# Attention output with the probabilities stationary instead of the values, in a fused attention and feed-forward kernel

## The chip, the cores and the metric

The program runs on one core of a Trainium2 chip. The metric is the device time of one execution in microseconds (us); lower is better. Three runs of the kernel before are given, and one more execution was taken by the hardware profiler.

## What is computed

The reference, cut to the part that the change touches; two feed-forward layers follow it (a layer norm, an up product to 2048 columns with relu, a down product back to 512 and a residual; then a mixing over tokens and the same again).

```python
batch, n_heads, seq, head_dim = (4, 8, 576, 64)
...
scores = scale * np.matmul(q, k.transpose(0, 1, 3, 2))
...
scores = np.where(causal, -1000000000.0, scores + np.minimum(bias, 0.0))
scores = scores - np.max(scores, axis=-1, keepdims=True)
attn = np.exp(scores)
attn = attn / (np.sum(attn, axis=-1, keepdims=True) + 1e-09)
return np.matmul(attn, v).astype(np.float32)
```

## The kernel before, in words

There are 32 heads (4 batches of 8), handled one after the other. The 576 queries of a head are 5 tiles of 128 rows, the last with 64; because of the causal mask tile i needs only the keys of tiles 0 to i. Every float32 operand of a product is held as a high and a low part, and the products of the parts are added up in PSUM.

For one head u the engines do this:

- TensorE transposes the loaded q, k and the last rows (L646 to L672), makes the scores of tile i (`scores`, L674), and transposes the probabilities of tile i, so that keys lie on partitions (`transpose_probs`, L696).
- VectorE adds the bias and takes the row maximum (L1141), ScalarE takes the exponential (L942). ScalarE then copies the transposed probabilities out as their high part (`probs_high`, L952), VectorE makes the low part (`probs_low`, L1156).
- GpSimd splits the values of the head into high and low halves that lie beside each other, 64 columns each, in `v2` (`split_values`, L574). It waits until TensorE is done with the values of the head before.
- `times_values` (L706) multiplies values and probabilities, one head late: in the turn of head u it works on head u-1. The values are stationary (128 columns: high and low half of each of the 64 value columns), the probabilities move. Part 0 covers queries 0 to 255 (4 matmuls), part 1 queries 256 to 575 (10 matmuls). The result lies in one bank, `ps_x`, with the 64 + 64 value columns on partitions. ScalarE copies the lower half out (`out_low`, L959), VectorE adds the halves (`out_sum`, L1163). Since the bank is shared, part 1 waits for the sum of part 0.
- `transpose_out` (L728) turns the sum back in 5 transposes, so that queries lie on partitions, and VectorE scales it by one over the row sum into `x_head` (`out_scale`, L1180). SyncE stores `x_head` to DRAM (`store_head`, L381).

The work comes in stages. Heads 0 to 10 run alone (`head_alone` on each engine; AHEAD is 11). After them 21 heads (11 to 31) run with blocks of the first feed-forward layer between their pieces: `head` with `fill(1)` to `fill(8)`, 4 heads to one block. The output of the last head is finished in the following quarter of a block (`last_output`). The rest of the span is feed-forward work alone.

The order on every engine is written out by hand; an engine runs its own list in order and waits on semaphores. Two lists matter here beside those above. On GpSimd, in the stage of the heads alone, `pair` (L589) has for every head u: `split_values`, then `split_weights` of weight pair u (L560, four operations of 128x512). On SyncE, `head_alone` (L394) has for every head u: the last rows of head u+2, the values of head u+1, the sums of head u+2, q of head u+3, `store_head` of head u-1, k of head u+3, and `next_weights` (L389), which loads weight pair u+1. There are two staging slots for weights, and pairs 0 and 1 are loaded ahead of the loop.

## Time and profile before

| | us |
|---|---|
| median of 3 runs | 1136.02 |
| lowest and highest of them | 1135.39, 1136.83 |
| span of the profiled execution (first to last instruction) | 1134.1 |

The profiled execution has no total time of its own beside its span; what lies around the span is at most the difference to the runs, 1.3 to 2.7 us. Instructions in the profile are named by engine, line of the kernel, and output and input tiles. PE is TensorE's matmuls and PEld its weight loads, DVE is VectorE, ACT ScalarE, POOL GpSimd, SP SyncE; SPq is SyncE issuing a DMA. Matmuls overlap, so what one costs in a stream is the distance from its start to the start of the next, and not its duration. In the stage of the heads alone some tiles share memory with others: `w_hi`, `w_lo` and `zt` in rows of L691, L723 and L1159 are the second buffers of the transposed probabilities and of q and k.

### The profile page before, as it was taken

The page shows a single profiled execution, that of the slowest core. Times are in us where ns is not written, and L with a number is a line of the kernel's source. Part 1 is how long each engine was busy: PE and PEld are TensorE (multiplying, and loading weights), DVE is VectorE, ACT ScalarE, POOL GpSimd, SP SyncE. Part 2 cuts the span into 40 slices and gives each one's busy share as a digit, 9 for nine tenths or more (in the row PEclk, how much of TensorE's full clock was granted, in tenths as well). Part 3 has the DMA queues.
Part 4 walks back from the last instruction along what each step waited for, and adds up shares of the span by engine and source line. Part 5 has one row for each costly group of instructions (what it writes and reads, how often), then busy time and mean ns, then how long its engine had stood idle before and what let it go on. Part 6 is the DMA issues. An engine that isn't in the chain of part 4 may idle for free.

```text
span 1134.1 us, 21431 instructions
## 1 busy us (share of the span) xinstructions
PE 1099.9 (97%) x7320; PEld 967.4 (85%) x7320; DVE 490.6 (43%) x1252; ACT 399.9 (35%) x1051; POOL 161.0 (14%) x183
## 2 busy tenths in 40 slices
PE   6887999999999999999999998999999999999998
PEld 5776888888888888889889787889898898898987
DVE  5999456566565565652231365321212212112121
ACT  5887445445454454441221244111111111111111
POOL 2776533010101010102100032000000000000000
PEclk9999999999999999999999999999999999999999
DMA  6667343313222323114301156003101101011010
GB/s 157 167 181 198 109 111 94 90 40 110 57 74 74 92 74 92 42 49 129 130 1 55 38 197 218 13 19 121 55 0 55 40 15 55 0 55 55 0 38 19
DMA packets 126184, 88.57 MB, mean 78 GB/s; under 512 B 87425, under 2 KB 99713, under 8 KB 126145
## 3 DMA queue, kind: packets, MB, share of 16 engines
q1 hardware_dynamic: 123584, 79.67, 23.9%
q0 software_dynamic: 2560, 8.39, 2.2%
q8 instruction: 23, 0.38, 0.1%
q14 instruction: 17, 0.13, 0.0%
HBM read 69.61 MB, written 18.42 MB: 78 GB/s over the span
## 4 chain that ended last, share of the span: by engine, by line
PE 91%; DMA 4%; SPq 2%; issue 1%; DVE 1%; ACT 1%; POOL 0%; DVEq 0%; ACTq 0%; POOLq 0%
PE ps_up L815 12%; PE ps_acc L832 12%; PE ps_up L816 12%; PE ps_up L817 11%; PE ps_acc L833 11%; PE ps_acc L834 11%; PE ps_x L723 4%; PE ps_s L691 4%; PE ps_pt L702 4%; DMA x_in<-u_dram 2%; PE ps_up L802 2%; PE ps_x L891 1%; DMA u_dram<-x_pair 1%; PE ps_x L733 1%; PE ps_x L653 1%
## 5 line engine op out<-in xcount | busy, mean ns | idle before, releaser
L815 PE MATMUL ps_up<-zt,w_hi 128*128 128x256 f32 x1152 | 333.2, 289 | 1.5 <-DVE zt L1273 1.0
L816 PE MATMUL ps_up<-zt,w_hi 128*128 128x256 f32 x1152 | 324.7, 282 | 0.0
L817 PE MATMUL ps_up<-zt,w_lo 128*128 128x256 f32 x1152 | 322.4, 280 | 0.0
L1278 DVE SCALAR_TENSOR_TENSOR h_lo<-ps_up,h_hi 128x256 fp32r<-128x256 f32 x288 | 122.2, 425 | 441.4 <-ACT h_hi L1029 440.8
L1029 ACT ACTIVATE h_hi<-ps_up 128x256 fp32r<-128x256 f32 x288 | 110.0, 382 | 494.1 <-PE ps_up L817 493.9
L832 PE MATMUL ps_acc<-w_hi,h_hi 128*128 128x512 f32 x576 | 237.1, 412 | 0.0
L815 PEld LDWEIGHTS ps_up<-zt,w_hi 128*128 128x128 f32 x1152 | 217.7, 189 | 15.0 <-DVE zt L1273 5.3
L833 PE MATMUL ps_acc<-w_lo,h_hi 128*128 128x512 f32 x576 | 227.1, 394 | 0.0
L834 PE MATMUL ps_acc<-w_hi,h_lo 128*128 128x512 f32 x576 | 227.1, 394 | 0.0
L816 PEld LDWEIGHTS ps_up<-zt,w_hi 128*128 128x128 f32 x1152 | 217.5, 189 | 7.4 <-issue 0.2
L817 PEld LDWEIGHTS ps_up<-zt,w_lo 128*128 128x128 f32 x1152 | 217.9, 189 | 0.0
L949 ACT ACTIVATE prob<-prob,neg_max 128x128 f32<-128x128 f32 (+4 forms) x160 | 96.8, 605 | 119.3 <-DVE neg_max L1152 119.3
L834 PEld LDWEIGHTS ps_acc<-w_hi,h_lo 128*128 128x128 f32 x576 | 108.4, 188 | 26.2
L832 PEld LDWEIGHTS ps_acc<-w_hi,h_hi 128*128 128x128 f32 x576 | 109.8, 191 | 13.3 <-issue 0.2
L833 PEld LDWEIGHTS ps_acc<-w_lo,h_hi 128*128 128x128 f32 x576 | 108.8, 189 | 13.9 <-issue 0.2
L1152 DVE CUSTOM_DVE_ANT_0 prob<-ps_s,ncum_b 128x128 f32<-128x128 f32 (+4 forms) x149 | 78.0, 524 | 52.4 <-PE ps_s L693 48.6
L702 PE MATMUL ps_pt<-ident_f,prob 128*128 128x128 f32 (+1 forms) x414 | 65.4, 266 | 11.4 <-ACT prob L949 11.4
L578 POOL TENSOR_TENSOR v<-v_raw,one 128x320 fp32r<-128x320 f32 x32 | 23.6, 737 | 284.6 <-PE ps_x L723 266.9
L1159 DVE TENSOR_TENSOR pt_lo<-ps_pt,pt_hi 128x128 fp32r<-128x128 f32 (+4 forms) x123 | 58.8, 478 | 7.2 <-ACT pt_hi L955 7.1
L955 ACT ACTIVATE pt_hi<-ps_pt 128x128 fp32r<-128x128 f32 (+4 forms) x123 | 52.9, 430 | 18.2 <-PE ps_pt L702 17.3
L702 PEld LDWEIGHTS ps_pt<-ident_f,prob 128*128 128x128 f32 (+1 forms) x414 | 41.0, 140 | 17.8 <-issue 12.9
L691 PE MATMUL ps_s<-k_hi,q 128*128 128x256 f32 (+4 forms) x146 | 51.8, 359 | 0.0
(138 smaller groups left out, 1209.0 us busy)
## 6 DMA issues: line engine op xcount, KB each, us to landing
ncum_b<-ncum_dram SPq DMA_DIRECT2D x32, 288.0 KB, 3.7
k_raw<-in_k SPq DMA_DIRECT2D x64, 128.0 KB, 2.7
stage<-in_moe_w_ch SPq DMA_DIRECT2D x32, 256.0 KB, 3.9
x_in<-x_dram SPq DMA_DIRECT2D x9, 512.0 KB, 3.6
x_res<-x_dram SPq DMA_DIRECT2D x9, 512.0 KB, 4.0
u_dram<-x_pair SPq DMA_DIRECT2D x2, 2304.0 KB, 10.9
x_in<-u_dram SPq DMA_DIRECT2D x9, 512.0 KB, 4.5
x_res<-u_dram SPq DMA_DIRECT2D x9, 512.0 KB, 3.7
```

The lines of the kernel that those rows point to most:

```text
L691: last = nc.tensor.matmul(bank, q2[:, i * P:(i + 1) * P], kk[:, lo:hi], start=(n == 0), stop=(n == 1 and not diag))
L702: last = nc.tensor.transpose(bank[:, c * r:(c + 1) * r], prob_of(p, i, alone)[0][0:r, c * P:(c + 1) * P], ident[0:r, 0:r])
L815: nc.tensor.matmul(up[j % 2][:, 0:BLK], w1_hi[:, j, c], zt_hi[:, c], start=(c == 0), stop=False)
L816: nc.tensor.matmul(up[j % 2][:, 0:BLK], w1_hi[:, j, c], zt_lo[:, c], start=False, stop=False)
L817: last = nc.tensor.matmul(up[j % 2][:, 0:BLK], w1_lo[:, j, c], zt_hi[:, c], start=False, stop=(c == KC - 1))
L832: nc.tensor.matmul(acc[t], h_hi[:, j % 2, cols], w2_hi[:, j], start=first, stop=False)
L833: nc.tensor.matmul(acc[t], h_hi[:, j % 2, cols], w2_lo[:, j], start=False, stop=False)
L834: last = nc.tensor.matmul(acc[t], h_lo[:, j % 2, cols], w2_hi[:, j], start=False, stop=final)
L949: nc.scalar.activation(at[:, 0:w], at[:, 0:w], ACT.Exp, bias=least, scale=-1.0, accum_out=row_sum[:, p, i:i + 1]).then_inc(exp_done, 1)
L1029: nc.scalar.activation(h_hi[:, j % 2], up[j % 2][:, 0:BLK], ACT.Relu).then_inc(L.h_hi_done, 1)
L1152: nc.vector.tensor_tensor_reduce(out=like(to[:, 0:w]), in0=scored, in1=like(ncum_b[p][:, 0:w]), scale=1.0, scalar=3.0e38, op0=ALU.add, op1 ...
L1278: nc.vector.scalar_tensor_tensor(out=h_lo[:, j % 2], in0=up[j % 2][:, 0:BLK], scalar=0.0, in1=h_hi[:, j % 2].bitcast(F32), op0=ALU.max, op ...
```

## The change

The two operands of the product change places. For query tile i and key tile c the transposed probabilities are stationary (`pt[:, c * ROW + i * P ...]`, 128 columns, 64 in the last tile) and the values move (128 columns). Tiles 0 to 2 are part 0, tiles 3 and 4 part 1. The queries now lie on partitions; VectorE adds the two halves, which lie beside each other in the free dimension, by `tensor_reduce` into `x_sum`, once in part 0 and twice in part 1; GpSimd scales `x_sum` into `x_head`. `out_low` and `transpose_out` are gone. GpSimd's list for a head u in the stage of the heads alone is now `split_values` (u), `split_weights` (u), `out_scale` (u-1); in the later heads it is `split_values` (u), `out_scale` (u-1), and then weights where there are any. The first `out_sum` of a head waits until the scaling of the head before is done with `x_sum`.

```diff
-PARTS = (0, 2 * P, S)
-MOST = max(PARTS[1], S - PARTS[1])
+OUT_TILES = ((0, 1, 2), (3, 4))
...
+            def out_scale(m, p):
+                u = 2 * m + p
+                pool.wait_ge(x_sum_done, 2 * u + 2)
+                pool.wait_ge(inv_done, u + 1)
+
+                waits_apart(pool, (x_stored, 32 * u))
+                pool.tensor_tensor(x_head[:], x_sum[:], inv_sum[:, p].unsqueeze(2).to_broadcast([P, QT, D]), ALU.mult)\
+                    .then_inc(x_head_done, 1)
...
                 for p in range(2):
                     split_values(m, p)
                     split_weights(2 * m + p, p, m)
+                    if not (isinstance(m, int) and m == 0 and p == 0):
+                        out_scale(*before(m, p))
...
                     split_values(*beside(n, i))
+                    out_scale(*before(*beside(n, i)))
                     for j in range(AHEAD + 2 * i, min(AHEAD + 2 * i + 2, JC)) if weights else ():
...
-                waits_apart(pe, (q_loaded, 16 * u + 16), (l_lo_done, u) if alone else (x_head_done, u - 1))
+                waits_apart(pe, (q_loaded, 16 * u + 16), (l_lo_done, u) if alone else (x_sum_done, 2 * (u - 1)))
...
-                begin, end = PARTS[a:a + 2]
-                tiles = -(-end // P)
-                for c in range(tiles):
-                    lo, hi = max(c * P, begin), end
-                    for pt in (pt_hi, pt_lo):
-                        last = nc.tensor.matmul(ps_x[:, lo - begin:end - begin], v2[:, c].rearrange("p a d -> p (a d)"),
-                                                pt[:, c * ROW + lo:c * ROW + hi], start=(c == 0 and pt is pt_hi),
-                                                stop=(c == tiles - 1 and pt is pt_lo))
-                last.then_inc(ot_done, 1)
-
-            def transpose_out(m, p):
...
+                wait(pe, x_sum_done, 2 * u + a)
+                for i in OUT_TILES[a]:
+                    r, at = rows(i), (i - OUT_TILES[a][0]) * P
+                    for c in range(i + 1):
+                        for pt in (pt_hi, pt_lo):
+                            last = nc.tensor.matmul(ps_x[0:r, at:at + P], pt[:, c * ROW + i * P:c * ROW + i * P + r],
+                                                    v2[:, c].rearrange("p a d -> p (a d)"), start=(c == 0 and pt is pt_hi),
+                                                    stop=(c == i and pt is pt_lo))
+                last.then_inc(out_done, 1)
...
-            def out_low(m, p, a):
-                act.wait_ge(ot_done, 2 * (2 * m + p) + a + 1)
-                n = PARTS[a + 1] - PARTS[a]
-                nc.scalar.activation(ot_low[:, 0:n], ps_x[D:2 * D, 0:n], ACT.Copy).then_inc(ot_low_done, 1)
...
             def out_sum(m, p, a):
                 u = 2 * m + p
-                dve.wait_ge(ot_low_done, 2 * u + a + 1)
+                dve.wait_ge(out_done, 2 * u + a + 1)
                 if a == 0:
 
-                    wait(dve, ox_done, u)
-                n = PARTS[a + 1] - PARTS[a]
-                nc.vector.tensor_tensor(ot_sum[:, PARTS[a]:PARTS[a + 1]], ps_x[0:D, 0:n], ot_low[:, 0:n], ALU.add)\
-                    .then_inc(ot_sum_done, 1)
+                    wait(dve, x_head_done, u)
+                first, n = OUT_TILES[a][0], len(OUT_TILES[a])
+                both = ps_x[:, 0:n * P].rearrange("p (t a d) -> p t d a", t=n, a=2)
+                if a == 0:
+                    last = nc.vector.tensor_reduce(x_sum[:, 0:n], both, mybir.AxisListType.X, ALU.add)
+                else:
+                    nc.vector.tensor_reduce(x_sum[:, first:QT - 1], both[:, 0:n - 1], mybir.AxisListType.X, ALU.add)
+                    last = nc.vector.tensor_reduce(x_sum[0:LAST, QT - 1:QT], both[0:LAST, n - 1:n], mybir.AxisListType.X, ALU.add)
+                last.then_inc(x_sum_done, 1)
...
-            def out_scale(m, p):
-                u = 2 * m + p
-                dve.wait_ge(ox_done, u + 1)
-                dve.wait_ge(inv_done, u + 1)
-
-                wait(dve, x_stored, 32 * u)
-                nc.vector.tensor_tensor(x_head[:], ps_x[:, 0:QT * D].rearrange("p (t d) -> p t d", d=D),
-                                        inv_sum[:, p].unsqueeze(2).to_broadcast([P, QT, D]), ALU.mult).then_inc(x_head_done, 1)
```

## Rows read from the trace of the kernel before

**Rows 1.** Windows: length, busy us of PE, PEld, DVE, ACT, POOL; clock, DMA, GB/s.

```profile
28.20:104.80 76.60, 66.25 (x543) 56.83 (x542) 72.08 (x218) 65.98 (x189) 55.63 (x54) 1.00 0.72 193
121.10:512.90 391.80, 391.78 (x2782) 343.63 (x2781) 229.66 (x632) 196.93 (x533) 60.76 (x67) 1.00 0.28 76
104.80:121.10 16.30, 11.62 (x76) 10.62 (x75) 10.10 (x28) 8.12 (x21) 7.26 (x7) 0.79 0.49 134
```

**Rows 2.** Timeline of PE, one later head: start, duration, line, tiles, shape.

```profile
284.85 0.36 PE L723 MATMUL ps_x<-pt_hi,v 128*128 128x256 f32 x1
...
285.34 0.45 PE L832 MATMUL ps_acc<-w_hi,h_hi 128*128 128x512 f32 x1
...
288.80 0.31 PE L723 MATMUL ps_x<-pt_hi,v 128*128 128x320 f32 x1
...
290.05 0.44 PE L702 MATMUL ps_pt<-ident_f,prob 128*128 128x128 f32 x2
...
292.08 0.40 PE L834 MATMUL ps_acc<-w_hi,h_lo 128*128 128x512 f32 x1
292.41 0.52 PE L733 MATMUL ps_x<-ident_f,ot_sum 64*128 64x64 f32 x5
292.86 0.55 PE L702 MATMUL ps_pt<-ident_f,prob 128*128 128x128 f32 x3
...
293.82 0.60 PE L653 MATMUL ps_x<-ident_f,q_raw 128*64 128x128 f32 x4
294.18 0.36 PE L815 MATMUL ps_up<-zt,w_hi 128*128 128x256 f32 x1
```

**Rows 3.** Timeline of PE's weight loads in the same head.

```profile
285.18 0.19 PEld L723 LDWEIGHTS ps_x<-pt_lo,v 128*128 128x128 f32 x1
285.29 0.19 PEld L832 LDWEIGHTS ps_acc<-w_hi,h_hi 128*128 128x128 f32 x1
```

**Rows 4.** Groups by line and shape: busy us, mean ns of one, idle before.

```profile
L578 POOL TENSOR_TENSOR v<-v_raw,one 128x320 fp32r<-128x320 f32 x32 | 23.6, 737 | 284.6 <-PE ps_x L723 266.9 <-DMA v_raw<-in_v 10.5 <-issue 7.2
...
L1152 DVE CUSTOM_DVE_ANT_0 prob<-ps_s,ncum_b 128x384 f32<-128x384 f32 x32 | 17.6, 550 | 0.0
...
L1186 DVE TENSOR_TENSOR x_head<-ps_x,inv_sum 128x320 f32<-128x320 f32 x32 | 15.6, 488 | 12.3 <-PE ps_x L733 12.3
L1170 DVE TENSOR_TENSOR ot_sum<-ps_x,ot_low 64x320 f32<-64x320 f32 x32 | 15.4, 481 | 15.2 <-ACT ot_low L962 15.0
...
L962 ACT ACTIVATE ot_low<-ps_x 64x320 f32<-64x320 f32 x32 | 13.9, 435 | 17.1 <-PE ps_x L723 16.5
```

**Rows 5.** Timeline of SP issuing, heads alone.

```profile
50.58 0.42 SPq L385 DMA_DIRECT2D x_dram<-x_head  x1
...
53.21 0.37 SPq L323 DMA_DIRECT2D stage<-in_moe_w_ch  x1
...
59.46 0.41 SPq L385 DMA_DIRECT2D x_dram<-x_head  x1
...
67.40 0.41 SPq L385 DMA_DIRECT2D x_dram<-x_head  x1
```

**Rows 6.** Waits of SP, 20 to 110 us: us in total, times, longest.

```profile
SPq L71 <- DVE x_head L1186: 0.4, 2, 0.2
```

**Rows 7.** Timeline of POOL, heads alone.

```profile
57.46 1.04 POOL L570 TENSOR_TENSOR w_hi<-stage,one 128x512 f32 x1 [2.33 <-DMA stage<-in_moe_w_ch]
...
62.45 0.72 POOL L578 TENSOR_TENSOR v<-v_raw,one 128x320 fp32r<-128x320 f32 x1
63.25 0.86 POOL L580 TENSOR_TENSOR v<-v_raw,v 128x320 fp32r<-128x320 f32 x1
```

**Rows 8.** Timelines of POOL and PE at the ends of the heads alone.

```profile
33.57 1.29 POOL L572 TENSOR_TENSOR w_lo<-stage,w_hi 128x512 fp32r<-128x512 f32 x1
...
104.52 0.28 PE L723 MATMUL ps_x<-w_lo,v 128*128 128x64 f32 x1
...
113.36 0.58 PE L815 MATMUL ps_up<-zt,w_hi 128*128 128x256 f32 x1 [0.96 <-DVE zt L1273]
```

More of the change, by code:

```diff
@@ L138, in chain_kernel @@
                               for name, w1 in (("pt_hi", w1_hi), ("pt_lo", w1_lo)))
-            ot_low = sbuf("ot_low", [D, MOST], F32, small)
-            ot_sum = sbuf("ot_sum", [D, SP_PAD], F32, small)
+            x_sum = sbuf("x_sum", [P, QT, D], F32, small)
             x_head = sbuf("x_head", [P, QT, D], F32, small)
@@ L609, in _ @@
             split_weights(AHEAD - 1, 0, AHEAD // 2)
+            out_scale(*before(AHEAD // 2, 0))
             group(0, weights=True)
@@ L613, in _ @@
             split_values(*LAST_HEAD)
+            out_scale(*before(*LAST_HEAD))
+            out_scale(*LAST_HEAD)
             pool.wait_ge(x_stored, 32 * HEADS)
@@ L712, in times_values @@
                     pe.wait_ge(v_split, u + 1)
-                    wait(pe, x_head_done, u)
-                else:
-                    pe.wait_ge(ot_sum_done, 2 * u + 1)
-                begin, end = PARTS[a:a + 2]
-                tiles = -(-end // P)
-                for c in range(tiles):
-                    lo, hi = max(c * P, begin), end
-                    for pt in (pt_hi, pt_lo):
-                        last = nc.tensor.matmul(ps_x[:, lo - begin:end - begin], v2[:, c].rearrange("p a d -> p (a d)"),
-                                                pt[:, c * ROW + lo:c * ROW + hi], start=(c == 0 and pt is pt_hi),
-                                                stop=(c == tiles - 1 and pt is pt_lo))
-                last.then_inc(ot_done, 1)
-            def transpose_out(m, p):
-                u = 2 * m + p
-                waits_apart(pe, (ot_sum_done, 2 * u + 2))
-                for t in range(QT):
-                    last = nc.tensor.transpose(ps_x[:, t * D:(t + 1) * D], ot_sum[:, t * P:(t + 1) * P], ident[0:D, 0:D])
-                last.then_inc(ox_done, 1)
+                    if not alone:
+                        pe.wait_ge(l_lo_done, u + 1)
+                wait(pe, x_sum_done, 2 * u + a)
[7 more added lines that the diff above has]
+                last.then_inc(out_done, 1)
             def head_alone(m, p, first=False, final=False):
@@ L752, in head_alone @@
                 transpose_probs(m, p, 3, True)
-                if not first:
-                    transpose_out(*before(m, p))
                 transpose_probs(m, p, 4, True)
@@ L773, in head @@
                 fill(4)
-                transpose_out(*before(m, p))
                 transpose_probs(m, p, 2, False)
@@ L858, in last_output @@
                     times_values(*LAST_HEAD, step, False)
-                else:
-                    transpose_out(*LAST_HEAD)
             def first_input():
@@ L957, in probs_high @@
                     .then_inc(pt_hi_done, 1)
-            def out_low(m, p, a):
-                act.wait_ge(ot_done, 2 * (2 * m + p) + a + 1)
-                n = PARTS[a + 1] - PARTS[a]
-                nc.scalar.activation(ot_low[:, 0:n], ps_x[D:2 * D, 0:n], ACT.Copy).then_inc(ot_low_done, 1)
             def head_alone(m, p, first=False, final=False):
                 probs_high(m, p, 0, True)
-                if not first:
-                    out_low(*before(m, p), 0)
                 exponential(m, p, 2, True)
@@ L971, in head_alone @@
                 exponential(m, p, 3, True)
-                if not first:
-                    out_low(*before(m, p), 1)
                 probs_high(m, p, 2, True)
@@ L992, in head @@
                 exponential(m, p, 1, False)
-                out_low(*before(m, p), 0)
                 fill(2)
@@ L997, in head @@
                 fill(3)
-                out_low(*before(m, p), 1)
                 probs_high(m, p, 1, False)
@@ L1062, in last_output @@
             def last_output(step):
-                if step < 2:
-                    out_low(*LAST_HEAD, step)
+                pass
             def scale_input():
@@ L1209, in head_alone @@
                 probs_low(m, p, 3, True)
-                if not first:
-                    out_scale(*before(m, p))
                 probs_low(m, p, 4, True)
@@ L1231, in head @@
                 fill(4)
-                out_scale(*before(m, p))
                 bias_and_max(m, p, 4, False)
@@ L1339, in last_output @@
                     out_sum(*LAST_HEAD, step)
-                else:
-                    out_scale(*LAST_HEAD)
             def split_input():
```

10 lines of the change are left out of this document (4 added, 6 removed).

## The prediction

> **What bounds the kernel now.** I read the windows by stage first [rows 1]. From 121.1 to 512.9 us, where heads and feed-forward blocks are mixed, TensorE has work in 391.78 of 391.80 us, and all other engines are idle 40% of the time or more. There a removed or added microsecond of TensorE's stream is one of the kernel, and what the change takes off ScalarE and VectorE is worth nothing. From 28.2 to 104.8 us the heads run alone. VectorE is busy for 72.1 of 76.6 us, TensorE for 66.3, GpSimd for 55.6, and no engine is the only bound.
>
> In that second stage I read the queue of SyncE next, because the change moves a step that it waits for. Its stores of a head's output start at 50.58, 59.46 and 67.40 us [rows 5], so two turns take 16.8 us, 8.4 us a head. It hardly ever waits: for `x_head` 0.4 us in 90 us [rows 6]. SyncE issues without a pause and sets the pace together with VectorE. GpSimd's list shows what hangs on SyncE: the split of a weight pair starts at 57.46 after 2.33 us of waiting for the load that SyncE issued at 53.21 [rows 5, 7], and lasts until 62.45, when the values of the next head follow at once. So GpSimd is full too, and late.
>
> **TensorE, later heads (22 of them: the outputs of heads 10 to 31).** Removed: part 0, 4 matmuls, from 284.85 to 285.34, 0.49 us; part 1, 10 matmuls, from 288.80 to 290.05, 1.25 us; the 5 transposes. The 512-column matmul ahead of them starts at 292.08, and one like it needs about 0.23 us (all of block work in this stage runs at that distance, an estimate from 6 of them between the rows), so the stream is free at 292.31 and goes on at 292.86: 0.55 us. Together 2.29 us [rows 2].
>
> Added: 12 matmuls in part 0 and 18 in part 1, 30 in all with 128 moving columns, each with a weight load of its own. Two loads of 128 columns start 0.11 us apart, at 285.18 and 285.29, where the matmuls between them have only 128 columns [rows 3]; so loading sets the distance, not moving, and 20 matmuls take 0.115 each (taking in the 0.12 that some pairs show), 2.3 us. The other 10 belong to the last query tile and load 64 columns. No row has such a load of this type. The nearest is the transposes of q, with 64-column loads: 4 in 0.36 us, 0.09 each [rows 2]. The ends are 0.06 (half of a full load) and 0.115 (as a full load); I take 0.09, 0.9 us. Sum 3.2 us against 2.29: +0.9 us a head, between +0.6 and +1.2. Times 22: **+20 us**, between +13 and +26.
>
> The Trainium skill, "TensorE: Matmul & The Clock Gate", section on LDWEIGHTS, says a load takes its number of columns over 1.2 ns, whatever the rows, which is against this change, since it multiplies loads. For the full loads the trace agrees (0.107 us stated, 0.11 measured). For the 64-column loads it would give 0.053 us and so +0.4 us a head, about +8 us in place of +20.
>
> **VectorE and ScalarE.** ScalarE loses both copies (the larger 435 ns). VectorE loses the scaling (488 ns) and two sums of about 0.45; it gains one reduction over 384 columns and two over 128. By the rows of the same input size a 384-column pass takes 0.55 us [rows 4]; the small ones I estimate at 0.28 each from the slope between 320 and 384 columns and these times' fixed part; sum 1.1 us against 1.4. If the stride of the reduction halves its speed it is 1.9 us. In the mixed stage both hide under TensorE. In the heads alone a gain of 0.3 us a head would be real, if nothing else grew.
>
> **GpSimd and SyncE, heads alone.** This is the larger term. Scaling a head costs GpSimd 0.74 us by the like operation on 128x320 [rows 4]; it might be 0.88, as the subtraction of that size (0.86 in rows 7). But it stands behind the whole weight split. In the turn of head u, SyncE waits at the store of head u-1 for this scaling; behind the store stand the loads of k and of weight pair u+1; GpSimd needs pair u+1 ahead of its next scaling. That closes a loop with one turn a head:
>
> - SyncE from store to weight load: 50.58 to 53.21, 2.6 us, 2.45 without the present crowding [rows 5];
> - issue to GpSimd's start: 53.21 to 57.46, 4.25 us [rows 5, 7]; with fewer transfers at a time (the DMA engines are 72% busy now, rows 1) I take 3.9;
> - the weight split, 57.46 to 62.45: 5.0 us [rows 7];
> - the scaling, 0.8 us, and two semaphore hops, 0.3 us together (estimate).
>
> Sum 12.45, taken as **12.5 us a head** where it is 8.4 today; 11.6 to 13.3 with the ends of its terms.
>
> A second loop is nearly as long. VectorE's first sum waits for the same scaling, since `x_sum` is one buffer; TensorE's part 1 waits for that sum, and GpSimd's next `split_values` waits for part 1. Reduction 0.55, part 1 about 1.8 (8 at 0.115, 10 at 0.09), values 1.66 (62.45 to 64.11 [rows 7]), weights 5.0, scaling 0.8, hops 0.3: 10.1 us. TensorE idles in each turn then, and after the idle time ahead of 110 us the window from 104.8 to 121.1 shows a mean clock of 0.79 [rows 1], so some of it ran at 1.2 GHz. At that level part 1 takes 3.6 us and this loop 11.9, still under 12.5. What waits with TensorE and VectorE there: everything of the next head, so nothing covers it.
>
> The number of turns: GpSimd's first scaling (head 0) follows the second weight pair, which ends at 34.9 now [rows 8]; with slower products ahead and 0.8 us of scaling I put it at 37. The scaling of head 8 is 8 turns later, at 137. Then comes part 1 for head 9: hop and reduction 0.7, part 1 2 to 3.6, so its end is at 140.5; today it is at 104.8 [rows 8]. The rest of the path to the first block product (113.36 now) is unchanged. **+35.5 us**, between +27 and +43. The scaling of head 9 comes about 14 us after that of head 8 and is needed by the second part in the next head only, after the block's first products; that cover is just enough, and if it is gone it costs 2 or 3 us.
>
> In the later heads there is no weight split between values and scaling, the scaling ends within 1 us of where it is now, and q's transposes wait for the sums alone. These waits I cost at nothing; the cover is the 15 us until the next head's part 0. In the first group scaling stands ahead of the weights, and the input loads of blocks, queued behind the stores, have several microseconds to spare (estimate).
>
> **Sum.** 1134.1 + 20 + 35.5 = 1189.6 us of span; the median of the runs lies 1.9 above the span, so **1191.5 us**.
>
> **Rivals.**
> 1. The store does not close the loop: weights arrive early enough, because SyncE passes the store in time or landing is quick. Then only the second loop counts, 10.1 us a head at the full clock: 8 turns of +1.7, 3 us at the ends, and +20: 1173 us. For it: GpSimd already waits for weights by only 1 to 2 us a head. Against: the store is ahead of the load in SyncE's list, without exception.
> 2. Neither loop binds, and the heads alone keep 8.4 us: 1156 to 1160 us. It would need the scaling to come out well before the weights; the diff puts it behind.
> 3. TensorE falls to 1.2 GHz for much of each turn, since it idles 3 to 4 us in each. Its stream, 66 us in 76.6 now, would lengthen a turn to about 14.5: +16, 1207 us.
> 4. Faster. The point is the distance of short matmuls in the later heads: if it is 0.06, because the chip loads the next operand under the last matmul, 30 take 1.8 us instead of 2.29, -11 us in 22 heads; and with VectorE's 0.3 us in 10 heads the kernel is at about 1122. It decides for the whole only if GpSimd's loops don't bind as well. Against: the load distance of 0.11 [rows 3], and the order of the lists. It turns over where the distance is under 0.076 us.
>
> **Chances.** Forecast 0.6, rival 1 0.16, rival 2 0.06, rival 3 0.13, rival 4 0.04, 0.01 for none of these. The range holds the forecast with its bounds (1176 to 1205), most of rival 1 and rival 3: 1168 to 1209. A measurement of this kernel can tell some 0.2% (2.3 us) from no change. Slower by more 0.95, within it 0.01, faster 0.04.
>
> **What would show it.** Right: from about 37 us on, GpSimd's scalings 12 to 13 us apart, a wait of SyncE for the scaling of 3 us or more in each turn, GpSimd waiting for weights some 4 us, TensorE idle ahead of part 1, and the first block product near 149 us; per later head 0.9 us more. Wrong: stores still 8.4 us apart (rival 2), GpSimd's wait gone and 10 us a head (rival 1), low clock through the stage (rival 3), or a distance of the new matmuls under 0.08 us (rival 4 and the lower end).

## The result and the profile after

The changed kernel takes **1176.36 us** (median of 4 runs, 1174.08 to 1177.33), beside 1135.8 for the kernel before (4 runs): ratio 1.0364 (95%: 1.0337 to 1.0390), 41 us slower. The profiled execution took 1174.08 us, its span 1172.4; it is the fastest of the four. The forecast was 1191.5 in 1168 to 1209: the sign and the range held, the size was 15 us too high.

The windows by stage of the changed kernel, the first from the split of the second head's values on, with the same columns as [rows 1]:

```profile
27.20:137.40 110.20, 87.53 (x652) 77.25 (x650) 72.16 (x223) 61.40 (x175) 61.60 (x63) 0.85 0.51 139
150.00:543.00 393.00, 392.98 (x2961) 352.16 (x2960) 222.82 (x625) 180.53 (x491) 76.97 (x88) 1.00 0.29 78
```

The stage of the heads alone has become much longer, and no engine is near to full in it. VectorE was busy for 72 of 77 us [rows 1]; now it is busy for 72 of 110. TensorE's granted clock there has fallen from 1.00 to 0.85. In the mixed stage TensorE is as full as it was.

Where the added time is, by the first block product, which answers to the last row of [rows 8]:

```profile
143.16 0.58 PE L814 MATMUL ps_up<-zt,w_hi 128*128 128x256 f32 x1 [0.96 <-DVE zt L1251]
```

It stood at 113.36 and stands at 143.16: 29.8 us of the 38.3 that the span has grown are spent before it, the other 8.5 in what follows.

**The loop of SyncE.** One turn, from the timelines of GpSimd and SyncE of the changed kernel [rows 5, 7]:

```profile
46.44 0.72 POOL L585 TENSOR_TENSOR x_head<-x_sum,inv_sum 128x320 f32<-128x320 f32 x1
...
53.59 1.04 POOL L567 TENSOR_TENSOR w_hi<-stage,one 128x512 f32 x1 [2.20 <-DMA stage<-in_moe_w_ch]
...
58.57 0.72 POOL L585 TENSOR_TENSOR x_head<-x_sum,inv_sum 128x320 f32<-128x320 f32 x1
```

```profile
47.37 0.42 SPq L382 DMA_DIRECT2D x_dram<-x_head  x1
...
49.98 0.37 SPq L320 DMA_DIRECT2D stage<-in_moe_w_ch  x1
```

The scaling ends at 47.16, the store is issued 0.2 us later, the weight load 2.6 us after the store, GpSimd starts on the weights 3.6 us after that (having stood for 2.2), splits them for 5.0 and scales the next head: 12.1 us from scaling to scaling. The ten scalings of the stage start between 33.80 and 145.55; the ninth is at 130.28, so eight turns take 96.5 us, 12.06 each, where the same eight took 68.3 (31.36 to 99.68), 8.5 each. In six of the eight (11.2 to 12.1 us) GpSimd waits for its weights, as above. In the other two, of 12.6 and 12.8 us, it does not; it waits 5.3 and 5.5 us for part 1 of TensorE, whose mean clock in these turns is 0.83 and 0.80. The second of them:

```profile
76.74 0.72 POOL L575 TENSOR_TENSOR v<-v_raw,one 128x320 fp32r<-128x320 f32 x1 [5.51 <-PE ps_x L733]
```

```profile
70.50:83.33 12.83, 11.30 (x81) 9.88 (x81) 7.81 (x24) 6.88 (x21) 6.82 (x8) 0.80 0.47 124
```

SyncE's waits between 25 and 140 us, and TensorE's, beside [rows 6]:

```profile
SPq L70 <- POOL x_head L585: 30.9, 9, 4.5
```

```profile
PE ps_pt L714 <- ACT prob L946: 15.3, 10, 1.5
PE ps_x L733 <- DVE x_sum L1157: 7.4, 5, 2.6
```

SyncE hardly waited for `x_head` before (0.4 us in two waits); now it does so nine times, 3.4 us on average and up to 4.5. TensorE stands ahead of part 1 five times, because VectorE's first sum waits for the scaling of the head before: the second loop of the prediction.

**A later head.** TensorE's timeline in one head of the mixed stage [rows 2]:

```profile
337.60 0.31 PE L733 MATMUL ps_x<-v,pt_hi 128*128 128x128 f32 x1
337.74 0.27 PE L733 MATMUL ps_x<-v,pt_lo 128*128 128x128 f32 x1
...
338.97 0.45 PE L831 MATMUL ps_acc<-w_hi,h_hi 128*128 128x512 f32 x1
...
342.42 0.22 PE L733 MATMUL ps_x<-v,pt_hi 128*128 128x128 f32 x1
...
343.26 0.22 PE L733 MATMUL ps_x<-v,pt_hi 128*64 128x128 f32 x1
343.33 0.22 PE L733 MATMUL ps_x<-v,pt_lo 128*64 128x128 f32 x1
...
343.87 0.40 PE L714 MATMUL ps_pt<-ident_f,prob 128*128 128x128 f32 x2
```

Part 0 takes 1.37 us (12 matmuls), part 1 1.45: 8 matmuls 0.105 apart, then 10 with 64 stationary columns 0.061 apart (343.26 to 343.87). Together 2.82 us against 2.29. Some of it is given back next to it. Four heads with their block, from one split of the values to the one four heads on, on GpSimd:

```profile
344.18 0.72 POOL L575 TENSOR_TENSOR v<-v_raw,one 128x320 fp32r<-128x320 f32 x1 [16.70 <-PE ps_x L733]
...
421.23 0.72 POOL L575 TENSOR_TENSOR v<-v_raw,one 128x320 fp32r<-128x320 f32 x1 [16.69 <-PE ps_x L733]
```

77.05 us; the same four heads took 75.32 before (290.36 to 365.68). That is 0.43 us a head.

VectorE and GpSimd, groups by shape of the changed kernel (columns as in [rows 4]):

```profile
L585 POOL TENSOR_TENSOR x_head<-x_sum,inv_sum 128x320 f32<-128x320 f32 x32 | 25.0, 782 | 13.9 <-DVE x_sum L1160 13.9
...
L1157 DVE TENSOR_REDUCE x_sum<-ps_x 128x192 f32<-128x384 f32 x32 | 17.8, 557 | 19.7 <-POOL x_head L585 10.1 <-PE ps_x L733 9.5
...
L1159 DVE TENSOR_REDUCE x_sum<-ps_x 128x64 f32<-128x128 f32 x32 | 9.3, 290 | 17.4 <-PE ps_x L733 17.4
L1160 DVE TENSOR_REDUCE x_sum<-ps_x 64x64 f32<-64x128 f32 x32 | 8.7, 273 | 0.0
```

The three reductions take 1.12 us a head, as forecast (1.1), the scaling 0.78 on average.

### The profile page after: what moved, and what is told of

Same layout as the page of the kernel before. It is cut to its first block, busy times and chain, and to the rows that moved or that the text cites. A ratio compares the mean times of both kernels' runs of the same rounds, so it can differ in the third digit from the quotient of the medians.

```text
span 1172.4 us, 22058 instructions
## 1 busy us (share of the span) xinstructions
PE 1127.7 (96%) x7672; PEld 1002.1 (85%) x7672; DVE 483.1 (41%) x1252; ACT 376.4 (32%) x987; POOL 184.5 (16%) x215
## 4 chain that ended last, share of the span: by engine, by line
PE 89%; DMA 4%; issue 2%; POOL 2%; SPq 1%; DVE 1%; ACT 1%; POOLq 0%; DVEq 0%; ACTq 0%
PE ps_up L814 12%; PE ps_up L815 11%; PE ps_acc L831 11%; PE ps_up L816 11%; PE ps_acc L832 11%; PE ps_acc L833 11%; PE ps_x L733 7%; PE ps_s L703 4%; PE ps_pt L714 3%; DMA x_in<-u_dram 2%; PE ps_up L801 1%; PE ps_x L888 1%; DMA stage<-in_moe_w_ch 1%; POOL w_hi L567 1%; DMA u_dram<-x_pair 1%
## 5 line engine op out<-in xcount | busy, mean ns | idle before, releaser
L814 PEld LDWEIGHTS ps_up<-zt,w_hi 128*128 128x128 f32 x1152 | 217.7, 189 | 14.5 <-DVE zt L1251 5.3
L946 ACT ACTIVATE prob<-prob,neg_max 128x128 f32<-128x128 f32 (+4 forms) x160 | 96.5, 603 | 129.4 <-DVE neg_max L1137 129.4
L733 PE MATMUL ps_x<-v,pt_hi 128*128 128x128 f32 (+1 forms) x405 | 82.7, 262 | 4.4 <-DVE x_sum L1157 4.4
L733 PE MATMUL ps_x<-v,pt_lo 128*128 128x128 f32 (+1 forms) x405 | 81.2, 261 | 0.0
L733 PEld LDWEIGHTS ps_x<-v,pt_hi 128*128 128x128 f32 (+1 forms) x405 | 70.4, 177 | 4.8 <-DVE x_sum L1157 4.8
```

Source lines behind the costliest of these rows:

```text
L733: last = nc.tensor.matmul(ps_x[0:r, at:at + P], pt[:, c * ROW + i * P:c * ROW + i * P + r], v2[:, c].rearrange("p a d -> p (a d)"), start= ...
L814: nc.tensor.matmul(up[j % 2][:, 0:BLK], w1_hi[:, j, c], zt_hi[:, c], start=(c == 0), stop=False)
L946: nc.scalar.activation(at[:, 0:w], at[:, 0:w], ACT.Exp, bias=least, scale=-1.0, accum_out=row_sum[:, p, i:i + 1]).then_inc(exp_done, 1)
```

## The experiments

The theory from here on: in the heads alone the scaling behind the weight split closes two loops, SyncE's (12.06 us a turn) and that of `x_sum` (about 10), and they make most of the 30 us there; the rest is the longer product. The rival: the loops only fill time that TensorE needs anyway. Ratios are to the kernel before, whose median was 1134.9 to 1135.5 in each set of runs; brackets hold the 95% interval. They are not the ratios of the two medians, and a difference of medians can be a few us from one of ratios. "Turn" is the distance between successive scalings on GpSimd (or of another step that comes once a head) in the heads alone.

### Cutting both loops: the scaling ahead of the weights

`e1_scale_first`, an edit of the changed kernel, in `pair` and likewise for head 10:

```diff
                     split_values(m, p)
-                    split_weights(2 * m + p, p, m)
                     if not (isinstance(m, int) and m == 0 and p == 0):
                         out_scale(*before(m, p))
+                    split_weights(2 * m + p, p, m)
```

> The changed kernel with one edit: in the stage of the heads alone GpSimd scales head u-1 before it splits weight pair u, not after. Theory (two loops through the weight split set the turn of 12.06 us): both loops lose the 5 us of the split, the turn goes back to what SyncE's issues and VectorE need, 8.4 to 8.9 us; the first block product is near 116 to 119 us instead of 143, and the kernel takes 1145 to 1151 us. Rival (the short matmuls at the lower clock, or GpSimd's total work, make the turn long): the amount of work on each engine is the same, so the turn stays near 12 us and the time above 1170 us.

Measured: **1165.97 us** (1158.10 to 1167.13), ratio 1.0253 (1.0210 to 1.0296). Neither side's numbers. The loops are gone: SyncE does not wait for `x_head` any more, and TensorE does not wait for `x_sum`. But only some turns got short. Four of them, windows from one split of the values to the next:

```profile
38.40:47.70 9.30, 7.77 (x73) 6.95 (x72) 7.58 (x25) 6.59 (x19) 6.80 (x8) 1.00 0.39 99
47.70:60.20 12.50, 10.97 (x73) 9.70 (x72) 8.22 (x27) 6.58 (x19) 6.85 (x8) 0.73 0.66 181
60.20:73.20 13.00, 11.47 (x72) 10.32 (x71) 7.79 (x25) 6.58 (x19) 6.79 (x7) 0.68 0.48 123
86.80:96.10 9.30, 7.77 (x73) 6.95 (x72) 7.18 (x23) 6.59 (x19) 6.81 (x7) 1.00 0.45 119
```

The same work (72 or 73 matmuls in the records, 19 operations of ScalarE) takes 9.3 us at a granted clock of 1.00 and 12.5 to 13.0 us at 0.73 and 0.68; GpSimd's and ScalarE's busy times are the same in both. Inside the second of these turns, in windows of 1 us:

```profile
49.00:50.00 1.00, 0.02 (x1) 0.00 (x0) 0.94 (x5) 0.95 (x2) 1.00 (x2) 1.00 1.06 341
50.00:51.00 1.00, 0.45 (x6) 0.42 (x6) 0.66 (x3) 0.78 (x4) 0.63 (x2) 1.00 0.50 139
51.00:52.00 1.00, 1.00 (x7) 0.94 (x6) 0.45 (x1) 0.59 (x2) 0.78 (x2) 0.65 0.64 146
52.00:53.00 1.00, 1.00 (x6) 0.65 (x5) 0.43 (x4) 0.45 (x1) 1.00 (x2) 0.50 0.46 156
...
57.00:58.00 1.00, 1.00 (x7) 1.00 (x6) 0.90 (x4) 0.51 (x4) 0.00 (x0) 0.50 1.03 337
58.00:59.00 1.00, 1.00 (x10) 0.93 (x10) 0.92 (x5) 0.81 (x3) 0.00 (x0) 0.93 0.16 59
```

TensorE stands still from 49.0 to 50.5, and about 1 us after it has gone on, its clock goes to one half (1.2 GHz) for some 7 us, in which it is always busy. What it stood for, from TensorE's timelines; first the run, one turn later, then the kernel before at the same place:

```profile
63.05 0.50 PE L714 MATMUL ps_pt<-ident_f,prob 64*128 64x64 f32 x5 [1.53 <-ACT prob L946]
```

```profile
63.56 0.52 PE L733 MATMUL ps_x<-ident_f,ot_sum 64*128 64x64 f32 x5
65.16 0.31 PE L702 MATMUL ps_pt<-ident_f,prob 64*128 64x64 f32 x2 [1.08 <-ACT prob L949]
```

Ahead of the last transposes of a head TensorE waits for the last exponential. The five transposes that the change removes stood in that very gap. Without them the gap is 1.53 us instead of 1.08. The same standstill stands in the turn at full clock (1.53 us ahead of 41.23), so it does not always end in the low clock. The times of the runs go with the clock too: the run at 1158.10 us has a mean clock of 0.989 over its span, the other three (1164.98 to 1167.13) 0.980. The profile thus has a third effect beside loops and product, and the next runs take them one by one.

### The loops one by one

`e2_weights_first` leaves GpSimd's list as changed and turns SyncE's order round, which opens SyncE's loop alone:

```diff
                 if not first:
-                    store_head(*before(m, p))
+                    next_weights(2 * m + p + 1, 1 - p)
                 if not final:
                     load_k(*after(m + 1, p))
                 if not first:
-                    next_weights(2 * m + p + 1, 1 - p)
+                    store_head(*before(m, p))
```

> The changed kernel with one edit: in the stage of the heads alone SyncE issues the next weight pair before the store of x_head, no longer behind it. That cuts the loop through SyncE alone. Theory (two loops of nearly the same length): GpSimd no longer waits for weights, but VectorE's first sum still waits for the scaling behind the split; the turn is the second loop's, 10.1 us at the full clock and more where TensorE has dropped to the lower one, so 10.2 to 11.9 us; the kernel takes 1158 to 1173 us. Rival 1 (the loop through SyncE is the only one): 8.4 to 8.9 us a turn, 1145 to 1151 us. Rival 2 (only the loop through VectorE counts): no change, 1174 to 1178 us.

Measured: 1163.34 us (1160.26 to 1166.46), ratio 1.0243 (1.0212 to 1.0275). The turns at full clock are the second loop's, by three scalings on GpSimd; 9.89 and 9.88 us, where the prediction's sum was 10.1:

```profile
35.69 0.72 POOL L585 TENSOR_TENSOR x_head<-x_sum,inv_sum 128x320 f32<-128x320 f32 x1
45.58 0.72 POOL L585 TENSOR_TENSOR x_head<-x_sum,inv_sum 128x320 f32<-128x320 f32 x1
55.46 0.72 POOL L585 TENSOR_TENSOR x_head<-x_sum,inv_sum 128x320 f32<-128x320 f32 x1
```

The other turns are 12.5 to 13.6 us at the low clock, as in the run before.

`e3_two_sums` opens the second loop alone: two buffers of `x_sum`, and the first sum waits for the scaling of two heads ago (so does the inverse of the row sums).

```diff
-                    wait(dve, x_head_done, u)
+                    wait(dve, x_head_done, u - 1)
+
+                x_sum = x_sums[p]
```

> The changed kernel with x_sum doubled, so that VectorE's first sum of head u waits for the scaling of head u-2 and not of u-1 (and the inverse of the row sums waits for the same, since it too would be overwritten). That cuts the loop through VectorE alone. Theory: the loop through SyncE stays, 2.6 + 3.6 + 5.0 + 0.7 + 0.2 = 12.1 us a turn; the time changes by less than 4 us, 1172 to 1177 us, and TensorE's idle time moves to where it waits for values. Rival (the loop through VectorE is the one that counts): 8.4 to 9.5 us a turn, 1145 to 1155 us.

Measured: 1173.59 us (1170.37 to 1177.39), ratio 1.0333 (1.0307 to 1.0360). SyncE still waits as in the changed kernel, and the last six turns of the stage are still 11.5 to 12.2 us (the first two, where GpSimd waits 6 us for TensorE at a mean clock of 0.63 and 0.80 and not for weights, take 13.3 and 13.5); VectorE's wait of `x_sum` for `x_head` is gone:

```profile
SPq L70 <- POOL x_head L585: 31.0, 9, 4.5
```

So SyncE's loop is the longer one, and opening the other moves the time by no more than the intervals allow (they overlap).

`e23_both` has both edits.

> Both edits together: the weight pair issued ahead of the store, and two buffers for x_sum; GpSimd's order as in the change, the scaling still behind the split. Theory: with both loops cut nothing ties the scaling to the next head; GpSimd's list of 7.4 us fits under SyncE's 8.3, so the turn is 8.4 to 9.0 us and the kernel takes 1145 to 1152 us, as in the run with the scaling moved ahead. Rival (GpSimd is simply too full with 0.73 us more): the turn stays over 10 us and the time over 1160 us.

Measured: 1163.79 us, ratio 1.0237 (1.0180 to 1.0294), from two runs at 1157.31 and 1158.20 (mean clock 0.987 and 0.989) and two at 1169.38 and 1169.44 (0.980 and 0.979). The profile is that of `e1_scale_first`: turns of 9.35 us or of 12.5 to 13.5. Both loops open in another way give the same as the scaling moved, and both miss what the loops alone would explain.

`e4_scale_dve` puts the scaling back on VectorE, at its place of before (between `probs_low` 3 and 4), and takes it off GpSimd; product and reductions stay changed.

```diff
                 probs_low(m, p, 3, True)
+                if not first:
+                    out_scale(*before(m, p))
                 probs_low(m, p, 4, True)
```

> The changed kernel with the scaling back on VectorE at its old place in the list, from x_sum; product and reductions as in the change. Both loops through the weight split are gone as in the run with the scaling moved ahead, and VectorE has 0.49 us more. Theory (what is left is TensorE's longer products in its own chain, and the clock): the same as that run, turns of 9.35 to 9.9 us at full clock and 12.5 and more at the lower, 1156 to 1169 us. Rival (GpSimd's part of the change is all that costs in this stage): 1145 to 1150 us.

Measured: 1165.82 us (1158.54 to 1167.78), ratio 1.0249 (1.0211 to 1.0288), turns of 9.3 to 9.9 or 12.5 to 13.9 us, much as in `e1_scale_first`. Who scales doesn't matter once the scaling does not stand behind the weights.

### The loop alone, on the kernel before

`e5_before_wait` is the kernel before with one wait more: in the heads alone SyncE waits at the store of head u-1 for GpSimd's weight split of pair u. Nothing of the product is changed.

```diff
                 if not first:
+                    waits_apart(sp, (layer_a.w2_split, 2 * m + p + 1))
                     store_head(*before(m, p))
```

> The kernel before with one wait added: in the stage of the heads alone SyncE stores head u-1 only when GpSimd has split weight pair u. No operation is added or longer. Theory (the loop through SyncE and the weight split alone makes a long turn): 0.2 + 2.6 + 3.6 to 4.2 + 5.0 us = 11.4 to 12.0 us a turn where it was 8.4, the first block product comes near 138 to 142 us instead of 113, and the kernel takes 1159 to 1166 us. Rival (the loop costs only together with the longer products): under 1145 us.

Measured: 1159.01 us (1156.89 to 1161.77), ratio 1.0200 (1.0183 to 1.0217). SyncE's and GpSimd's waits between 25 and 140 us:

```profile
SPq L71 <- POOL w_lo L573: 27.4, 9, 3.8
```

```profile
POOL w_hi L571 <- DMA stage<-in_moe_w_ch: 31.7, 8, 4.9
```

The loop by itself costs 23 us of the kernel before, with turns of 11.4 us (its stores start at 46.28 and, seven turns later, at 125.85): the order store, weight load, split closes it, whatever TensorE multiplies. The mean clock of its stage is 0.83, so this run too holds what the clock may cost. And it fell here although the product is the old one and no work of TensorE was removed. TensorE's waits for the last exponential are as short as before (at most 1.1 us); what is new are waits for loaded operands, up to 2.0 us for the keys and one of 3.0 for the last rows:

```profile
PE ps_up L665 <- DMA k_raw<-in_k: 6.6, 6, 2.0
```

### The clock

`e6_filler` is `e1_scale_first` with five transposes of an identity matrix back in the gap (into `ps_x`, read by nobody):

```diff
+            def filler(m, p):
+                waits_apart(pe, (x_sum_done, 2 * (2 * m + p) + 2))
+                for t in range(QT):
+                    nc.tensor.transpose(ps_x[:, t * D:(t + 1) * D], ident_f[0:D, 0:P], ident[0:D, 0:D])
...
                 transpose_probs(m, p, 3, True)
+                if not first:
+                    filler(*before(m, p))
                 transpose_probs(m, p, 4, True)
```

> The run with the scaling moved ahead of the split, and in the stage of the heads alone five transposes more a head, of the identity, where transpose_out stood; their output is not used, nothing else is changed. That run had turns of 9.35 us with a granted clock of 1.00 and turns of 12.5 to 13.6 us with 0.68 to 0.73. Theory (the clock falls because TensorE now stands still in the wait for the last exponential, 1.53 us where it was 1.08, since the transposes that filled it are gone): the idle time is back at 1.08 us, the clock stays at 1.00 and every turn takes 9.35 us; the kernel takes 1149 to 1155 us, the first block product comes near 123 us. Rival (the short matmuls, each as long as its weight load, are what the clock falls with): the clock still falls in about half of the turns, 1158 to 1168 us.

Measured: **1153.17 us** (1150.79 to 1156.34), ratio 1.0164 (1.0144 to 1.0184): adding work to TensorE takes 13 us off the median (10 by the ratios). Two turns, and TensorE's waits of the stage:

```profile
47.20:56.50 9.30, 8.22 (x78) 7.34 (x76) 7.52 (x25) 6.53 (x20) 6.82 (x8) 1.00 0.75 208
56.50:65.90 9.40, 8.32 (x79) 7.42 (x78) 7.68 (x25) 6.66 (x20) 6.90 (x8) 1.00 0.68 167
```

```profile
PE ps_pt L714 <- ACT prob L953: 10.5, 10, 1.1
```

78 matmuls in a turn instead of 73, the longest wait 1.1 us instead of 1.5, and every turn 9.35 us. This profile is of the fastest run (mean clock 0.995); the others have 0.990 to 0.994, so the clock was not quite as good in each.

It also shows what sets the 9.35 us. TensorE is busy for 8.27 us of a turn and waits 1.08 for the last exponential, and that is all of it. The kernel before was in the same position: of its 76.6 us TensorE is busy for 66.3 [rows 1] and waits 9.1 in this gap and 1.1 elsewhere, so it had no other slack there, and its shortest turns are 7.25 + 1.08 = 8.33 us:

```profile
PE ps_pt L702 <- ACT prob L949: 9.1, 9, 1.1
```

In such a head the old parts 0 and 1 take 0.49 and 1.33 us (from 41.28 and from 43.34 in the kernel before) and the new ones 1.39 and 1.52 (from 50.78 and from 53.73 in this run), 1.09 more; the turn grew from 8.33 to 9.35, 1.02. The removed transposes give nothing back there, since they stood in the gap, where TensorE waits anyway.

`e7_after_filler` puts the same filler into the changed kernel, where the loops are closed.

> The changed kernel as it is, GpSimd's order too, with the five idle transposes a head in the heads alone (their output is not used). Theory (two costs in this stage: the loops through the weight split set a turn of 10 to 12 us whatever the clock, and the clock adds only where TensorE is on the path): the loops stay, TensorE still waits 2 to 3 us a turn for the first sum, so the turn stays at 11.5 to 12.1 us and the kernel takes 1168 to 1176 us. Rival (the clock alone makes the difference to the run with the scaling moved ahead): 1152 to 1158 us, as with the filler there.

Measured: 1176.35 us (1171.86 to 1178.59), ratio 1.0343 (1.0316 to 1.0371), the changed kernel's time. The clock of the stage rises from 0.85 to 0.93, and TensorE waits longer ahead of part 1, 13.5 us where it was 7.4:

```profile
27.20:137.40 110.20, 86.30 (x718) 76.11 (x717) 73.10 (x229) 61.64 (x180) 61.65 (x63) 0.93 0.48 134
```

```profile
PE ps_x L733 <- DVE x_sum L1164: 13.5, 8, 2.6
```

GpSimd now waits for its weights in all eight turns, which take 95.2 us where they took 96.5. While SyncE's loop sets the turn, a faster TensorE buys next to nothing; the clock costs most where the loops are open.

`e8_before_gap` goes the other way: the kernel before with one of the five transposes of `transpose_out` in the heads alone. The outputs of query tiles 1 to 4 of those heads are left out.

```diff
                 if not first:
-                    transpose_out(*before(m, p))
+                    transpose_out(*before(m, p), 1)
```

> The kernel before, where the heads alone transpose only the first of the five tiles of the output back (the rest of x_head is left out there), so that TensorE stands still about 0.36 us longer in each wait for the last exponential; no product is changed. Theory of the gap: the clock falls in part of the turns in this kernel too, its mean in the stage goes under 0.9 and the time rises to 1140 to 1155 us. Rival (the short matmuls bring the clock down): the clock stays at 1.00, the turns at 8.4 us, and the time within 1132 to 1137 us.

Measured: 1138.91 us (1133.35 to 1142.12), ratio 1.0029 (1.0011 to 1.0047), between the two sides' intervals and just under that of the theory. With a longest wait of 1.3 us the clock falls in some turns, where it was 1.00 in all of the stage [rows 1]:

```profile
29.13:38.86 9.73, 8.40 (x58) 7.12 (x57) 8.16 (x25) 7.22 (x22) 5.93 (x7) 0.82 0.57 157
...
48.70:57.15 8.45, 7.12 (x58) 6.18 (x58) 7.76 (x26) 7.29 (x23) 5.52 (x6) 1.00 0.69 185
```

These windows run from scaling to scaling. Three of the eight turns have a clock of 0.82 or 0.83 and take 9.5 to 9.8 us, the five at 1.00 take 8.4 to 8.9. So such a turn costs about 1 us, and the three together make the 3 us of this run.

### The product alone

`e11_hybrid` is the kernel before with the new product and the reductions in the later heads only; the heads alone are as they were, and VectorE scales in both.

```diff
+                if not alone:
+                    for i in OUT_TILES[a]:
...
+                                last = nc.tensor.matmul(ps_x[0:r, at:at + P], pt[:, c * ROW + i * P:c * ROW + i * P + r],
+                                                        v2[:, c].rearrange("p a d -> p (a d)"), start=(c == 0 and pt is pt_hi),
+                                                        stop=(c == i and pt is pt_lo))
...
                 fill(4)
-                transpose_out(*before(m, p))
                 transpose_probs(m, p, 2, False)
```

> The kernel before in the heads alone, and the changed product with its reductions in the later heads only (22 outputs), the scaling on VectorE. Theory (there TensorE alone is the bound, and a head's new product costs 2.82 us against 2.24 to 2.29 for the old one with its transposes, of which blocks of four heads show 0.43 us each): 0.43 x 22 = +9.5 us, 1143 to 1146 us, four heads in 77.05 us instead of 75.33. Rival (the stage gains something from the engines relieved, or the 8.5 us between the first block product and the end come from elsewhere): under 1140 or over 1149 us.

Measured: 1143.92 us (1143.07 to 1150.24), ratio 1.0083 (1.0058 to 1.0108): 9 us, and they are the product of the later heads. The stage of the heads alone is that of [rows 1], at a clock of 1.00.

### Can the clock be had for the kernel before?

Between the last head alone and the first block product the kernel before has a mean clock of 0.79 [rows 1]. `e9_before_bridge` puts ten matmuls of 512 columns, on operands that are there, into TensorE's standstill in it:

```diff
+                pe.wait_ge(biased_done, QT * AHEAD)
+                pe.wait_ge(layer_a.w2_split, 1)
+                for _ in range(10):
+                    nc.tensor.matmul(acc[0], w1_hi[:, 0, 0], w2_hi[:, 0], start=True, stop=True)
                 pe.wait_ge(l_lo_done, AHEAD + 1)
```

> The kernel before with ten 512-column matmuls more, ahead of the first block's transposes, where TensorE stands still from 107.65 to 110.31 us for the normalised input; they write a bank that is started anew later, so nothing that is computed changes. Theory (the lower clock after that idle time, from 111.6 to 117.6 us, is paid on the path): the clock stays at the higher level, half of those 6 us is saved, less some tenths for the filler's end: 1131.5 to 1133.5 us against 1135.2, so a version that beats both. Rival (the products there are hidden behind VectorE and ScalarE, or the clock falls anyway): within 1 us of the kernel before.

Measured: 1134.16 us (1130.27 to 1138.32), ratio 0.9988 (0.9971 to 1.0005): not told apart from the kernel before. The window that had 0.79, and the filler and the products in it:

```profile
104.80:121.10 16.30, 14.04 (x100) 11.97 (x100) 11.30 (x33) 9.23 (x24) 8.12 (x9) 1.00 0.52 147
```

```profile
108.89 2.56 PE L867 MATMUL ps_acc<-w_hi 128*128 128x512 f32 x10
...
114.27 0.39 PE L815 MATMUL ps_up<-zt,w_hi 128*128 128x256 f32 x1 [1.03 <-DVE zt L1277]
114.50 0.28 PE L816 MATMUL ps_up<-zt,w_hi 128*128 128x256 f32 x1
114.62 0.28 PE L817 MATMUL ps_up<-zt,w_lo 128*128 128x256 f32 x1
```

The clock is kept, and the products follow each other 0.12 us apart instead of 0.21. In this execution the end of the heads alone was 1.3 us later than before (the last transposes at 108.47, not 107.17), and the first product only 0.9 later. Eleven such distances are another microsecond. So a gain of a microsecond or two can be read from the profile; but the median lies above the 1131.5 to 1133.5 us of the theory, and the runs cannot tell a gain from none.

`e10_filler_bridge` has that bridge on top of `e6_filler`.

> The run with the scaling moved ahead and the idle transposes, with the same ten matmuls ahead of the first block. Theory: the same gain on top of 1153.2 us, 1149 to 1152 us, the granted clock 1.00 from the first block on. Rival: no change, 1152 to 1155 us.

Measured: 1149.88 us (1147.42 to 1150.89), ratio 1.0127 (1.0105 to 1.0148), some 3 us under `e6_filler`; the intervals touch. It is the best form found of the changed product in all heads, and it is 14 us slower than the kernel before.

## Why the prediction was right, and where its sizes were off

The 41 us come apart as follows, by ratios times 1135.5:

| part | from | us |
|---|---|---|
| longer product in the later heads | `e11_hybrid` | 9 |
| longer product in the heads alone | `e6_filler` less `e11_hybrid`, 1.0164 - 1.0083 | 9 |
| loops through the weight split | changed kernel less `e6_filler`, 1.0364 - 1.0164 | 23 |

Each line has an interval of 3 to 4 us to either side, from those of its ratios. The profiles give much the same: the first block product of `e6_filler` is 6.9 us later than that of the kernel before (120.24 for 113.36), that of the changed kernel 22.9 later still.

The third line is not free of the clock: the changed kernel with the filler is at 1.0343, which makes the loops 20 us. With both loops open and no filler the clock takes 10 of them back (1.0253 - 1.0164), so that opening the loops alone shows only 13 of the 23.

**SyncE's loop: right.** It was forecast at 12.5 us a turn; the mean of the eight is 12.06, and 11.84 in the six turns that it sets. By its terms in the turn shown: store to weight load 2.6 (2.45 to 2.6 forecast), weight load to GpSimd's start 3.6 (3.9), split 5.0 (5.0), scaling and hops 0.9 (1.1). The forecast signs stand in the profile: SyncE's waits, GpSimd's for its weights (in six turns, up to 2.2 us and not the 4 forecast), TensorE idle ahead of part 1. They decide, and not the time: 1176.4 us is nearer to the 1173 of rival 1 than to the 1191.5 of the forecast, and rival 1's loop of 10.1 us a turn is what the profile does not show. `e5_before_wait` shows that the loop alone costs this on the old product. Rivals 1 and 2 fall with it.

**The second loop: right,** 9.9 us for 10.1 forecast, shown by `e2_weights_first` as the one that binds when SyncE's is open.

**First block product: 5.7 us too late.** 149 was forecast, 143.16 came. Eight turns at 0.44 us too much make 3.5. The rest is the start: the 37 of the prediction holds the 0.8 us of the first scaling, so it is its end, and that is at 34.53. The weights ahead of it were done at 33.8 (34.9 before) and not later than before, as forecast. This is the luck of one execution. In it the clock is 1.00 from 20 to 30 us, where the kernel before has 0.70 from 20 to 25. In the profiles of `e3_two_sums` and `e7_after_filler`, whose work is nearly the same up to there, it is 0.61 and 0.58 from 25 to 30 us, and the first scaling starts at 37.35 and 37.63. Their first block products are at 146.30 and 145.78.

**The step that was mis-sized is the later heads' product:** +0.9 us a head taken, between 0.6 and 1.2; +0.43 measured, below the lower end, so for this term the stated bounds did not hold. The 20 full loads went as forecast (0.105 to 0.115 us apart), the 10 loads of 64 columns are 0.061 apart and not 0.09. The price came from transposes with 64-column loads, which I took as the nearest row; they are no measure of the load. That is 0.3 of the 0.5 us. Of the remaining 0.2 the full loads make 0.1 (20 in 2.21 us, for 2.3 forecast) and the neighbours 0.1, which they give back (2.82 less 2.29 is 0.53 in the product itself, 0.43 in the turn). 22 heads at 0.43 make 9 us for 20.

The Trainium skill, "TensorE: Matmul & The Clock Gate", section on LDWEIGHTS, gives 0.053 us for 64 columns, where the trace shows 0.061, and 0.107 for 128, where it shows 0.105 to 0.115. The +8 us that the prediction worked out beside its sum by that rule is close to the 9 that came.

**What the prediction did not have:** the longer product in the heads alone. It was costed at nothing there, since SyncE and VectorE were said to set the pace. That reading was wrong: TensorE had no slack but its wait for the last exponential (see `e6_filler`), and VectorE's 72 busy us of 76.6 did not make it the bound. With the loops open and the clock at 1.00 the turn is 9.35 us, not 8.4, although SyncE and VectorE have less to do than before (VectorE is busy for 7.5 us of 9.3). TensorE's two parts and its wait for the last exponential are in the chain of a turn, and the 1.09 us by which the parts grew there stand beside 1.02 of the turn; with rival 2 this would have been 9 us short. It stayed unseen in the result, because SyncE's loop is longer still.

**Rival 3,** the clock, was half right. The clock does fall in the changed kernel (0.85), and for more than one reason: with the gap filled again it is still 0.93 (`e7_after_filler`), and with the loop alone on the old product 0.83 (`e5_before_wait`), so the idle time of the loops is one, as rival 3 had it, and the gap that the removed transposes had filled is another. But the turns did not go to 14.5 us. Six are set by the loop through SyncE, the DMA and GpSimd; two are TensorE's at the low clock and 0.5 to 1 us longer than the loop would make them. `e7_after_filler`, without such turns, takes the same time within its interval. **Rival 4** asked for a mean distance below 0.076 us; it is 2.82 / 30 = 0.094.

Left open: how much the short load-bound matmuls add to the fall of the clock. They are not needed for it: `e8_before_gap` lengthens the gap with the old product and has the clock fall in some turns, `e5_before_wait` makes TensorE wait elsewhere, with the old product and all of its work, and has it fall too; `e6_filler` has the new product and a clock of 1.00. But no run lengthened this very gap without removing TensorE work, and no run shows why the same standstill is followed by the low clock in one turn and not in the next.

## What to carry to other kernels

Before moving a step to an idle engine, follow who waits for its result in the queues: here 0.8 us of work put behind a 5 us weight split closed a loop through a DMA queue and cost 20 to 23 us, with GpSimd at work for only 56% of the stage. Swapping the operands so that each matmul moves fewer columns has its price in loads, one for each matmul; count them by their columns and compare with the moving columns that they replace. Count removed transposes only where TensorE has no wait that they stood in: here they took 0.55 us of the stream in a later head, and nothing was gained by their removal in a head alone. When TensorE work is removed from a stage where it waits, read the granted clock of that stage: work that looks like overhead may hold it.

## What was not expected of the hardware

- After a standstill of TensorE of 1.53 us the clock went from 1.00 to 0.50 for some 7 us in some turns and stayed in others of the same run, with the same instructions (9.3 us at 1.00, 12.5 to 13.0 at 0.73 and 0.68). In the profiles whose longest wait in the heads alone is 1.1 us it stayed (the kernel before from 28 us on, `e6_filler`); between 20 and 28 us the kernel before has one wait of 1.5 us and a mean clock of 0.79; with waits of up to 1.3 it fell in some turns (`e8_before_gap`).
- So runs of one such kernel lie apart: `e23_both` has two at 1157 to 1158 and two at 1169 us, with mean clocks of 0.987 to 0.989 and 0.979 to 0.980. A program whose clock behaves so needs more runs than one whose clock does not.
- Five transposes without use, about 0.5 us of TensorE's time in each head alone, made a kernel 10 to 13 us faster (1165.97 to 1153.17 by the medians, 1.0253 to 1.0164 by the ratios).
